# Summing raw rows of q, k and v on TensorE in an attention and feed-forward kernel

## The reference

```python
q_d = q.reshape(B, H, Sd, 4, D).mean(axis=3)        # likewise k_d, v_d
out_d = softmax(q_d @ k_d^T / 8) @ v_d              # pooled attention, 144 x 144 a head
out_up = repeat(out_d, 4, axis=2)
out_local = softmax(banded q @ k^T / 8) @ v         # |i - j| < 4
x = (out_up + out_local)  as 2304 x 512
x = rms_norm(x) * rms_g
x = (silu(x @ w_gate) * (x @ w_val)) @ w_out        # 512 -> 1536 -> 512
out = (s * relu(x @ w_in)^2 + b) @ w_out2           # 512 -> 2048 -> 512
```

## Time and profile before

| | |
|---|---|
| time, median of 3 runs | 980.24 us (979.86 to 981.27) |
| time of the profiled execution | 984.85 us |
| its span, first to last instruction | 982.9 us |
| TensorE busy | 949.1 us (97%) |
| VectorE busy | 537.4 us (55%) |
| ScalarE busy | 354.0 us (36%) |
| GpSimd busy | 368.4 us (37%) |
| mean granted TensorE clock | 0.978 |

### The profile page before, as it was taken

The page is one execution under the profiler, slowest core; times in us unless marked ns, Lnnn a source line. Parts: engine busy times, 40 slices in busy tenths (PEclk is TensorE's granted clock), DMA queues, the critical chain, the costliest instruction groups (busy, mean ns, idle before and its releaser), DMA issues.

```text
span 982.9 us, 13208 instructions
## 1 busy us (share of the span) xinstructions
PE 949.1 (97%) x5008; PEld 766.3 (78%) x5031; DVE 537.4 (55%) x813; ACT 354.0 (36%) x816; POOL 368.4 (37%) x192
## 2 busy tenths in 40 slices
PE   7888899989999999999999999999999999999998
PEld 4677699756777777777778998888888888888897
DVE  6888997886775765564542224444433443343343
ACT  2448854752324232422241444222322322222232
POOL 4757866777783876465600454000000000000000
PEclk9898799999999999999999999999999999999999
DMA  9898673433331331012003341102001100100010
GB/s 244 217 259 253 180 216 94 147 87 104 97 111 35 86 106 48 15 38 70 19 9 120 130 129 64 43 1 86 1 1 43 43 0 1 65 1 1 1 43 22
DMA packets 54379, 79.42 MB, mean 81 GB/s; under 512 B 9836, under 2 KB 37068, under 8 KB 52908
## 3 DMA queue, kind: packets, MB, share of 16 engines
q1 hardware_dynamic: 52284, 71.53, 24.8%
q10 hardware_dynamic: 2032, 7.05, 1.9%
HBM read 67.05 MB, written 11.50 MB: 80 GB/s over the span
## 4 chain that ended last, share of the span: by engine, by line
PE 78%; DVE 6%; DMA 4%; POOL 3%; ACT 3%; issue 2%; SPq 2%; ACTq 0%; DVEq 0%; POOLq 0%
PE bank L782 23%; PE bank L922 7%; PE bank L923 7%; PE bank L924 7%; PE bank L905 7%; PE bank L906 7%; PE bank L904 7%; PE bank L818 4%; PE bank L816 4%; PE bank L817 4%; POOL prod L551 3%; DMA rawv<-in_v_dram 2%; ACT prod_a L578 1%; DMA vs<-in_v_dram 1%; PE bank L726 1%
## 5 line engine op out<-in xcount | busy, mean ns | idle before, releaser
L551 POOL TENSOR_TENSOR prod<-qs,ks 128x896 f32<-128x896 f32 x80 | 177.7, 2244 | 89.7 <-DVE sc L596 62.9
L565 POOL TENSOR_TENSOR prod<-sc,vs 128x896 f32<-128x896 f32 x72 | 136.7, 2001 | 64.8 <-DVE x L606 32.7
L945 DVE SCALAR_TENSOR_TENSOR r<-bank,r 128x512 f32<-128x512 f32 (+1 forms) x80 | 51.1, 638 | 181.0 <-ACT r L933 181.0
L906 PE MATMUL bank<-y_h,w2i_l 128*128 128x512 f32 (+1 forms) x320 | 117.7, 368 | 0.0
L933 ACT ACTIVATE r<-bank 128x512 f32<-128x512 f32 (+1 forms) x80 | 44.4, 555 | 181.9 <-PE bank L906 181.2
L838 DVE TENSOR_TENSOR bank<-bank,u 128x512 f32<-128x512 f32 (+1 forms) x66 | 39.6, 599 | 118.0 <-PE bank L782 113.0
L782 PE MATMUL bank<-x_h,wv_h 128*128 128x512 f32 (+1 forms) x264 | 100.0, 390 | 0.0
L596 DVE TENSOR_REDUCE sc<-prod 128x14 f32<-128x896 f32 x80 | 85.7, 1078 | 18.0 <-POOL prod L551 18.0
L816 PE MATMUL bank<-h_h,wo_h 128*128 128x512 f32 (+1 forms) x264 | 93.1, 353 | 0.0
L818 PE MATMUL bank<-h_h,wo_l 128*128 128x512 f32 (+1 forms) x264 | 92.6, 351 | 0.0
L817 PE MATMUL bank<-h_l,wo_h 128*128 128x512 f32 (+1 forms) x264 | 92.5, 351 | 0.0
(11 more groups left out here) (142 smaller groups left out, 1935.7 us busy)
## 6 DMA issues: line engine op xcount, KB each, us to landing
raww<-in_moe_w_out_dram SPq DMA_DIRECT2D x14, 512.0 KB, 4.1
ks<-in_k_dram SPq DMA_DIRECT2D x16, 280.0 KB
vs<-in_v_dram SPq DMA_DIRECT2D x16, 280.0 KB, 5.0
y_scr<-y_st ACTq DMA_DIRECT2D x4, 1024.0 KB, 5.7
raww<-in_moe_w_in_dram SPq DMA_DIRECT2D x8, 512.0 KB, 3.5
y_raw<-y_scr SPq DMA_DIRECT2D x4, 1024.0 KB, 4.8
out_dram<-o_st SPq DMA_DIRECT2D x16, 256.0 KB, 2.8
rawq<-in_q_dram SPq DMA_DIRECT2D x3, 1152.0 KB, 15.2
```

The lines of the kernel that those rows point to most:

```text
L551: pool.tensor_tensor(dst, qv, kv, ALU.mult).then_inc(prod_ready, 1)
L565: pool.tensor_tensor(dst, pv, vv, ALU.mult).then_inc(prod_ready, 1)
L906: last = pe.matmul(o, w2i_l[:, m, kk, :], y_h[t % 2][:, kk, 0:w], start=False, stop=kk == DT - 1)
```

## The change

**q and k of batches 1 to 3.** VectorE's first addition is gone. TensorE now sums all four raw rows: four matmuls with `is_transpose` for each block in place of two, so 12 in a unit in place of six.

**v, all batches.** A batch has two more units, `("v", 0)` and `("v", 1)`, each for four heads: four float32 matmuls of 512 columns with the identity (72 x 72) as the stationary operand and the raw rows of v as the moving one, summed in PSUM. ScalarE copies the result straight to `dv`. VectorE's sums of v, the store of the sums and the load back are gone. The raw v of batches 1 to 3 is loaded in two halves to two places on 72 partitions; a half of batches 2 and 3 waits until the same unit of the batch before is done.

**Placement.** A batch now has eight units: v of batch 0 at the ends of turns 2 and 3, and batches 1 to 3 at the ends of turns 4 to 11, 12 to 19 and 20 to 27. The fillers stay.

**Products.** Tile 1's first two k products and their reductions stand before tile 0's v products. The v windows of tile 0 have eight places (`vs3` holds four more), so none of them waits for another.

**Queues.** The order of SyncE's queue and the places of single instructions on VectorE and ScalarE change; `weight_lo(1)` on VectorE moves from ahead of `least(29)` to behind `least(30)`.

```diff
-UNIT = [("q", 0), ("q", 1), ("k", 0), ("k", 1), ("q", 2), ("k", 2)]
+UNIT = [("q", 0), ("q", 1), ("k", 0), ("k", 1), ("v", 0), ("q", 2), ("k", 2), ("v", 1)]
+QK0 = 6
-UNIT_FROM = {1: 5, 2: 4, 3: 4}
+UNIT_FROM = 4
 def slot_units(n):
...
+    if n in (2, 3):
+        return ((0, QK0 + n - 2),)
+    b, i = divmod(n - UNIT_FROM, UNITS)
+    return ((b + 1, i),) if 0 <= b < B - 1 else ()
...
             def load_rawq(b):
                 if b == B - 1:
-                    sp.wait_ge(v0_pooled, 2)
+                    sp.wait_ge(ctr_ps, UNITS)
...
+            def load_rawv(b, g):
+                rows = v_rows[b][:, H * g:H * (g + 1), :]
+                if b == 0:
+                    sp.dma_start(rawv0[0:JH, H * g:H * (g + 1), :], rows).then_inc(rawv0_loaded[g], 16)
+                    return
+                if b > 1:
+                    sp.wait_ge(ctr_ps, UNITS * (b - 1) + UNIT.index(("v", g)) + 1)
+                sp.dma_start(rawv[1 + g][0:JH, :, :], rows).then_inc(rawv_loaded[g], 16)
...
             load_qk(sp, 0, 0)
-            load_rawv0(0)
+            load_rawv(0, 0)
+            load_qk(sp, 0, 1)
             load_rawq(1)
-            load_qk(sp, 0, 1)
+            load_rawv(0, 1)
             load_qk(sp, 0, 2)
-            load_rawv0(1)
             load_rawk(1)
...
             load_qk(sp, 0, 7)
-            load_rawv(2)
+            load_rawv(2, 0)
+            load_rawv(2, 1)
             load_v(sp, 0, 0)
+            load_v(sp, 0, 1)
+            load_qk(sp, 1, 0)
+            load_rawq(3)
...
             qk_mult(pool, 0, 15)
+            qk_mult(pool, 1, 0)
+            qk_mult(pool, 1, 1)
             pv_mult(pool, 0, 0)
...
+                if kind == "v":
+                    wait(act, cpv, H * (b - 1))
+                    act.activation(dv[0:JH, b % 2, H * g:H * (g + 1), :], CTR[0:JH, :].rearrange("p (h d) -> p h d", d=D), ACT.Copy).then_inc(ctr_evac, 1)
+                    return
...
             least(16)
             qk_reduce(dve, 0, 14)
             exponent_sums(1, 1)
             qk_reduce(dve, 0, 15)
             softmax_max(dve, 0)
             least(17)
+            qk_reduce(dve, 1, 0)
             softmax_norm(dve, 0)
-            pool_q(3)
+            qk_reduce(dve, 1, 1)
...
             add_pooled0(dve, 1)
-            weight_lo(dve, 1)
             least(29)
             inverse_root0(dve)
             least(30)
-            qk_reduce(dve, 1, 0)
+            weight_lo(dve, 1)
...
+                if kind == "v":
+                    if b == 0:
+                        pe.wait_ge(rawv0_loaded[g], 16)
+                    else:
+                        pe.wait_ge(rawv_loaded[g], 16 * b)
+                    pe.wait_ge(ctr_evac, n)
+                    rows = rawv0[0:JH, H * g:H * (g + 1), :] if b == 0 else rawv[1 + g][0:JH, :, :]
+                    for f in range(FAC):
+                        last = pe.matmul(CTR[0:JH, :], ident[0:JH, 0:JH], rows[:, :, f * D:(f + 1) * D], start=f == 0, stop=f == FAC - 1)
+                    last.then_inc(ctr_ps, 1)
+                    return
...
-                        for half in range(2):
-                            last = pe.matmul(to, raw[:, half * D:(half + 1) * D], ident[:, :], start=half == 0, stop=half == 1, is_transpose=True)
+                        for f in range(FAC):
+                            last = pe.matmul(to, raw[:, f * D:(f + 1) * D], ident[:, :], start=f == 0, stop=f == FAC - 1, is_transpose=True)
```

More of the change, by code:

```diff
@@ L69 @@
 ACT_PV = {0: (2, 6, 10, 13), 1: (2, 6, 10, 13)}
-PRODUCTS = [("qk", 0, n) for n in range(16)] + [("pv", 0, n) for n in range(16) if n not in ACT_PV[0]] + [("qk", 1, n) for n in range(16)]
+PRODUCTS = [("qk", 0, n) for n in range(16)] + [("qk", 1, 0), ("qk", 1, 1)]
+PRODUCTS += [("pv", 0, n) for n in range(16) if n not in ACT_PV[0]] + [("qk", 1, n) for n in range(2, 16)]
 EARLY = {2: 2, 3: 4, 4: 4}
@@ L240, in build @@
         at = [gl_start]
-        rawv = [None] + [place(at, f"rawv{b}", [P, QT, FAC * D], F32) for b in (1, 3)]
+        rawv = [None] + [place(at, f"rawv{g}", [P, H, FAC * D], F32) for g in range(2)]
+        at = [gl_start + 2 * QT * FAC * D * 4]
         vs2 = place(at, "vs2", [P, 2, WIN * D], F32)
@@ L244, in build @@
         at = [wo_start]
+        vs3 = place(at, "vs3", [P, H - WSLOTS0, WIN * D], F32)
         cs = place(at, "cs", [P, 4, 2 * J], F32)
@@ L304, in build @@
         rawv0_loaded = [sem(f"rawv0_loaded{g}") for g in range(2)]
[L305 to L310, removed]
+        q0_pooled, k0_pooled = sem("q0_pooled"), sem("k0_pooled")
+        rawv_loaded = [sem(f"rawv_loaded{g}") for g in range(2)]
+        k_order = sem("k_order")
         ctr_ps, ctr_evac = sem("ctr_ps"), sem("ctr_evac")
@@ L319, in build @@
         qk_loaded = [sem(f"qk_loaded{i}") for i in range(WSLOTS0)]
-        v_loaded = [sem(f"v_loaded{i}") for i in range(WSLOTS0)]
+        v_loaded = [sem(f"v_loaded{h}") for h in range(H)]
         prod_ready, prod_used = sem("prod_ready"), sem("prod_used")
@@ L494, in before_in_slot, with v_turn, v_before @@
             return (0, h + WSLOTS0) if a == 1 else (a - 1, h + H - 2)
+        def v_turn(a, h):
+            return 1 if a == 0 else 1 + (H // 2) * (a - 1) + h // 2 + 1
+        def v_before(a, h):
+            if a == 0:
+                return None
+            if h >= 2:
+                return (a, h - 2)
+            return (0, h) if a == 1 else (a - 1, h + H - 2)
         def q_win(a, h):
@@ L520, in load_v @@
         def load_v(sp, a, h):
-            last = before_in_slot(a, h)
+            last = v_before(a, h)
             if last is not None:
@@ L1265, in exponents @@
                                    accum_out=csum[0:JH, b % 2, 2 * h + a, 0:1]).then_inc(cexp, 1)
-            for i in range(UNITS):
+            for i in range(QK0):
                 keep_pooled(0, i)
@@ L1322, in _ @@
             exponents(18)
+            keep_pooled(2, 6)
             keep_turned(17)
             exponents(19)
+            keep_pooled(2, 7)
             keep_turned(18)
```

144 lines of the change are left out of this document (45 added, 99 removed).

## The result

The changed kernel takes 1012.86 us (median of four runs, 1010.24 to 1017.27) against 980.75 for the kernel before beside it: ratio 1.0327, 95% interval 1.0284 to 1.0371. The forecast was 993.0 in a range of 984 to 1001. The direction is right, the size is not: +32 us in place of +12.8. The profiled execution of after is its fastest, 1010.24 us with a span of 1008.4 and a mean granted clock of 0.988; against the profiled execution of before that is +25.5 us of span, and that difference is the one that can be followed in the traces. So of the 19 us beyond the forecast, 12.7 (25.5 - 12.8) can be followed there.

What follows compares the result with a forecast made beforehand. Engines around TensorE bound the head loop before; TensorE was to bound it after. The first gate 14.3 us later, less 1.5 us given back towards tile 1, made +12.8 us: 980.24 + 12.8 = 993.0 us, range 984 to 1001.

Steps and rivals of the forecast that it cites:

- Prices of the units: TensorE's head loop: a v unit 3.4 us, a q or k unit 1.31, a turn without a unit 1.69.
- Rival 1: V units: float32 columns pass as fast as bf16, 0.9 us a unit; kernel faster, some 975.5 us; chance 0.08.
- TensorE takes over as the bound: Head loop: TensorE's work becomes 112 us at full clock without waits, ending at 125.8 against today's 122.7.
- The wait for v at turn 3: End of turn 3: TensorE waits some 4 us for batch 0's second half of raw v, landing at 28.0 us.
- From there the loop has work without a gap ... I count no wait in them: Turns 4 to 27: 88.9 us of TensorE work without waits, so turn 28 starts at 120.3.
- From turn 28 to the first gate: Transposes of x 9.4 us after turn 28 starts (0.9 + 8.5), the first gate 7.3 later, at 137.0.
- "1.5 us" given back: First gate to tile 1's x: 1.5 us shorter, for VectorE subtractions no longer meeting GpSimd; bounds 0 and 6.2.
- Rival 2: Way to tile 1's x gives back 6.2 us in place of 1.5; 988.3 us; chance 0.14.
- the three signs that the prediction had named for being wrong: V units under 1.4 us, loop waits over 5 us after turn 4, or first gate to TensorE's last wait shrinking over 6.
- Rival 4: No net change: loop without any wait ends 3.1 us later, 1 to 5 given back; about 980 us; chance 0.04.
- Rival 3: Head loop: clock falls in the wait for v, more waits follow, costing up to 7 us; 1000 us; chance 0.12.
- after the wait of 4 us there is only work: Argument against low clock in the head loop: no gaps between waits, only work after turn 3's wait of 4 us.

Runs made afterwards that it cites:

- a_wlo1: Changed kernel with the weight subtraction `weight_lo(1)` on VectorE back in its old place ahead of `least(29)`: 1012.92 us, ratio 1.0323.
- d_cover07: Changed kernel with eight filler matmuls ahead of unit (0,7), which waits for its half of v at turn 3: 1004.47 us, ratio 1.0244.
- a_nowait: a_rawv with ScalarE's exponents of head 18 and copy of unit (2,6) ahead of the second pair of band products of (0,2): 994.53 us, ratio 1.0139.
- a_rawv: Changed kernel with the second half of batch 0's raw v loaded right behind the first half: 1002.20 us, ratio 1.0223.
- d_cover27: a_rawv with eight filler matmuls ahead of unit (2,7) in turn 19, where TensorE waited for ScalarE's copy: 998.46 us, ratio 1.0175.
- b_qk4: Kernel before with only the q and k part: TensorE sums raw rows of batches 1 to 3, VectorE's half sums left out: 980.15 us, ratio 0.9994.
- n_qk2: a_nowait with q and k halved on VectorE again, so only the v part of the change: 998.07 us, ratio 1.0157.
- n_vone: a_nowait with one of the four products in each v unit, three of v's four rows left out: 983.44 us, ratio 1.0002.
- a_both: Changed kernel with `weight_lo(1)` back ahead of `least(29)` and the second half of batch 0's raw v loaded earlier: 1005.59 us, ratio 1.0245.

## Why the prediction was wrong

- **Prices of the units: right.** 3.44, 1.31 and 1.70 us, as forecast. Rival 1 (float32 columns as fast as bf16) is refuted.
- **TensorE takes over as the bound: right.** It is busy 22.00 of 22.00 and 23.00 of 23.00 us from 38 to 83.
- **The wait for v at turn 3: there, size wrong the other way.** Landing by 24.8, not 28.0, in the profile (26.6 in a_wlo1's, with the same loads in the same order). My landing time, from bytes at the mean rate behind head 2's windows, was 3.2 us too late.
- **"From there the loop has work without a gap ... I count no wait in them": this is the step that failed.** I priced 88.9 us for turns 4 to 27 at full clock. They took 127.32 - 31.03 = 96.3, and the unit ahead of them 2.8 more than its price. Some 3.7 us of turn 4, a part of turn 5 and those 2.8 are low clock behind one wait of 1.8 us, which d_cover07 gives back by filling it. Of the 3.4 us of excess behind turn 5, 2.2 are short stops behind ScalarE (1.7 us at 94.32, 0.4 at 106), whose copies stand behind its band products; for the last 1.3 the profile has no stop, so the prices of the turns were a little low in sum. I had looked at ScalarE's share of time between two units of a bank, and not at what stands ahead of `keep_pooled(2, 6)` in its order. In a_nowait, with the longest of these stops away, turns 4 to 27 take 91.3 us (26.23 to 117.52), 2.4 over their price, 1.1 of it in short stops.
- **From turn 28 to the first gate: right.** Transposes 136.80 - 127.32 = 9.5 us on (forecast 9.4), the gate 5.9 further (7.3): 1.3 us less than forecast in all.
- **From the first gate on, "1.5 us" given back: a second step that failed, wrong in sign.** TensorE's last wait ends 114.5 us after the first gate against 108.2 before. 3.7 us are the wait for u behind weight piece 4, whose load the moved `weight_lo(1)` held back, and 1.7 us are a later wait for another subtraction of weights (`wv_l`). I had counted that move as a gain of 1.8 us only and had not asked what SyncE's queue has behind it. a_wlo1, with the subtraction moved back, shortens this way by 5.5 us and loses 3.2 of it ahead of the first gate. Rival 2, which had 6.2 us given back here, is refuted: the way is 6.3 us longer.
- **The sum.** Against the forecast, the profile has -3.2 us (landing of v), +2.8 (the unit behind it), +7.4 (turns 4 to 27), -1.3 (turn 28 to the first gate) and +7.8 (the way to tile 1): +13.5 at 257.21. None of the three signs that the prediction had named for being wrong came up.
- **Rival 4 (no net change)** is refuted by the ratio of 1.0327.
- **Rival 3 (1000 us, 0.12) named the mechanism,** with one more stretch of low clock. I spoke against it with "after the wait of 4 us there is only work". In after and in a_rawv's turn 19, the clock stayed low through some 14 and 12 us of just such dense work. The Trainium skill ("TensorE: Matmul & The Clock Gate", section "What's actually happening") has it that activity releases the throttled default state. I had drawn from that, that a denser loop keeps its clock; the 24 to 38 us stretch, busy 13.20 of 14.00 at 0.55, speaks against it here. The price of up to 7 us for one such stretch is about right (8.1 in d_cover07, 4.7 in d_cover27), but there was more than one place for it.
- **What of the loss is which part.** By b_qk4 and n_qk2 the q and k part is free; by n_vone the three added products a v unit are worth 13.4 us, all of what a_nowait loses. The remaining 18 us of the changed kernel went with two edits, to the load order (10.2) and to ScalarE's order (8.2).

How far each profiled execution stands for its kernel is limited: after's wait at 94.32 had no low clock behind it, and the same wait had it in the profiles of a_rawv, a_both, a_wlo1 and d_cover07. Why one stop is followed by low clock and another of the same length is not stays open.

## What to carry to other kernels

When work is moved onto an engine until it is the bound, price its stops again: look at every place where it waits in order for a load or for an in-order neighbour, since each now costs its length and, on TensorE, possibly a long stretch at half clock behind it. Moving the load and the neighbour's one instruction was worth more here (18 us) than taking three quarters of the v products away (13.4); where it can't be moved, fillers over the wait kept the clock in two runs. Where TensorE was not the bound, neither its added work (11.7 us in b_qk4) nor its clock showed in the time.

## What the runs showed of the hardware

- A wait of 1.7 to 1.8 us in front of dense work was followed by 12 to 14 us at a mean granted clock of 0.55 to 0.57, with TensorE busy at least 94% of it (after from 24 us, a_rawv from 85 us). Fillers over the same wait left it at 1.00, twice (d_cover07, d_cover27). It did not follow every such wait: in after the clock was 1.00 behind the 1.72 us at 94.32.
- A float32 product of 512 columns took 0.86 us of issue (3.44 us for four, eight records). In a q or k unit the float32 transposes of 128 columns took 0.109 us each (1.31 us for twelve), one record each, so half as much a column (0.85 against 1.68 ns).
- Mostly at the low clock the v unit took 6.23 us against 3.44, 1.8 times. The q unit behind it, all at the low clock, took 2.56 us (35.98 to 38.54) against 1.31, 1.95 times.
